# Attention and two MLPs on one Trainium2 core: the projections of queries and keys as one float32 matmul per half head

## What is computed

```python
q_bits = (einsum('bhsd,dk->bhsk', q, proj) > 0)      # proj: 64 x 6
k_bits = (einsum('bhsd,dk->bhsk', k, proj) > 0)
mask = bucket(q_bits)[:, :, :, None] == bucket(k_bits)[:, :, None, :]
scores = where(mask, q @ k.T / 8, -1e9)
x = softmax(scores) @ v                              # 1536 x 512 after the heads are joined
g = s * relu(x @ w_in) ** 2 + b                      # 512 -> 2048
x = g @ w_out
out = ((x @ w1) * (x @ w2) @ w3) @ w_out2            # 512 -> 1024 -> 512
```

## Time and profile before

| | |
|---|---|
| median of three runs | 818.06 us |
| the profiled execution | 818.39 us |
| its span | 816.5 us |
| PE busy | 778.7 us, 95% |
| DVE busy | 481.5 us, 59% |
| ACT busy | 383.7 us, 47% |
| POOL busy | 232.4 us, 28% |
| attention | until about 303 us |
| granted TensorE clock | 1.00 throughout |

### The profile page before, as it was taken

How to read it: one execution, slowest core, us unless ns; L and a number is a source line. 1 busy time by engine, 2 the same in 40 slices (tenths; PEclk the granted TensorE clock), 3 DMA queues, 4 the chain that set the end, 5 groups by cost and what they waited for, 6 DMA issues and landing times.

```text
span 816.5 us, 11692 instructions
## 1 busy us (share of the span) xinstructions
PE 778.7 (95%) x3776; PEld 632.6 (77%) x3776; DVE 481.5 (59%) x838; ACT 383.7 (47%) x718; POOL 232.4 (28%) x150
## 2 busy tenths in 40 slices
PE   3999999999989879999999999999999999999998
PEld 2787778777777768888888888888887888888886
DVE  4899999999989961156665656656576211210220
ACT  2788889888889963344231232323143211211221
POOL 3345555545565454563220211202022000000000
PEclk9999999999999999999999999999999999999999
DMA  5342223232242122233110101101010000001001
GB/s 147 75 97 62 64 61 80 79 81 63 61 119 71 44 78 65 90 103 104 52 51 1 52 0 51 51 1 51 1 53 0 1 26 26 1 14 39 0 0 51
DMA packets 14095, 42.17 MB, mean 52 GB/s; under 512 B 2386, under 2 KB 4434, under 8 KB 14066
## 3 DMA queue, kind: packets, MB, share of 16 engines
q1 hardware_dynamic: 14066, 41.79, 17.9%
HBM read 34.61 MB, written 3.15 MB: 46 GB/s over the span
## 4 chain that ended last, share of the span: by engine, by line
PE 73%; DVE 11%; issue 7%; ACT 5%; DMA 1%; DVEq 0%; SPq 0%; POOL 0%; ACTq 0%
PE psum L984 53%; PE psum L1071 8%; DVE top L728 4%; PE psum L910 3%; PE psum L923 3%; DVE pt_lo L742 3%; ACT prob L501 2%; PE psum L899 2%; PE psum L893 2%; ACT pt_hi L524 1%; DVE x_lo L846 1%; DVE exp_at L735 1%; DMA stage<-in_w_out 1%; PE psum L884 1%; DVE qm L721 1%
## 5 line engine op out<-in xcount | busy, mean ns | idle before, releaser
L501 ACT ACTIVATE prob<-psum,exp_at 128x768 f32<-128x768 f32 x96 | 96.5, 1005 | 29.8 <-DVE exp_at L735 29.8
L742 DVE TENSOR_TENSOR pt_lo<-psum,pt_hi 128x384 fp32r<-128x384 f32 x192 | 98.1, 552 | 11.1 <-ACT pt_hi L524 9.6
L728 DVE TENSOR_REDUCE top<-psum 128x1 f32<-128x768 f32 x96 | 91.0, 948 | 4.3 <-PE psum L899 4.0
L618 ACT ACTIVATE relu<-psum 128x512 f32<-128x512 f32 x48 | 28.6, 597 | 137.3 <-PE psum L984 137.3
L910 PE MATMUL psum<-ident,prob 128*128 128x128 f32 x576 | 85.1, 281 | 7.3 <-DVE pt_lo L742 6.9
L984 PE MATMUL psum<-x_hi,w_c 128*128 128x512 f32 (+1 forms) x288 | 90.6, 396 | 0.0
L984 PE MATMUL psum<-x_hi,w_b 128*128 128x512 f32 (+1 forms) x288 | 90.6, 396 | 0.0
L524 ACT ACTIVATE pt_hi<-psum 128x384 fp32r<-128x384 f32 x192 | 84.2, 495 | 11.0 <-PE psum L910 10.1
L869 DVE TENSOR_TENSOR ab<-psum,a_sb 128x512 f32<-128x512 f32 x24 | 16.6, 692 | 121.3 <-ACT a_sb L668 121.3
L823 DVE SCALAR_TENSOR_TENSOR relu<-psum,relu 128x512 f32<-128x512 f32 x48 | 33.1, 690 | 87.8 <-ACT relu L618 82.7
L910 PEld LDWEIGHTS psum<-ident,prob 128*128 128x128 f32 x576 | 65.4, 141 | 22.1 <-DVE pt_lo L742 13.2
(11 more groups left out here) (92 smaller groups left out, 1516.7 us busy)
## 6 DMA issues: line engine op xcount, KB each, us to landing
raw<-in_qk SPq DMA_DIRECT2D x30, 384.0 KB, 5.0
stage<-in_w_out SPq DMA_DIRECT2D x12, 512.0 KB, 3.4
stage<-in_w3t SPq DMA_DIRECT2D x8, 512.0 KB, 3.2
stage<-in_w_in SPq DMA_DIRECT2D x8, 512.0 KB, 3.3
stage<-in_w SPq DMA_DIRECT2D x8, 512.0 KB, 3.2
raw_v<-in_v SPq DMA_DIRECT2D x16, 192.0 KB, 2.6
qm<-both_hi SPq DMA_DIRECT2D x16, 192.0 KB, 2.7
out<-out_sb SPq DMA_DIRECT2D x12, 256.0 KB, 2.0
```

The costliest lines, as they stand in the source:

```text
L501: act.activation(prob[:, t % 3], score[t % 2], ACT.Exp, bias=exp_at[:, t % 2, 1:2], scale=exp_at[:, t % 2, 0:1], accum_out=rsum[:, (t // 3 ...
L728: dve.tensor_reduce(top[:, t % 2, 1:2], score[t % 2], AX.X, ALU.max, negate=True).then_inc(top_done, 1)
L742: dve.tensor_tensor(pt_lo[at], turned[part].rearrange("p (j q) -> p j q", j=3), pt_hi[at].bitcast(F32), ALU.subtract).then_inc(pt_lo_done, 1)
```

## The change

Queries and keys are loaded a third time, without any scaling or rounding: `qk_f` holds q of a head in its lower 64 partitions and k in its upper 64, two DMAs of 192 KB a head, two heads in turn. `pw` becomes one 128 x 128 float32 matrix, with proj in the rows of q at the columns 64 and 76, and in the rows of k at the columns 96 and 102, where the four rounded ones had it. `dots` is then one plain float32 matmul of 128 rows, 128 columns and 384 positions. It waits for the load instead of q_lo and k_lo; the waits for these two move to the first scores of a head. At the start proj comes first, as two DMAs, then `qk_f` of head 0, and `pw` is four copies on DVE ahead of the scale of head 0; `pj_hi` and `pj_lo` go. `qk_f` of head h + 3 is loaded behind `copy_bits` of head h + 1. The scratch space for DMA descriptors is set to 1024 bytes, which makes room in SBUF.

```diff
-            pw = sb("pw", [P, 4, P], FR, a)
-            pj_lo = sb("pj_lo", [P, BITS], FR, a)
-            pj_hi = sb("pj_hi", [P, BITS], FR, a)
+            pw = sb("pw", [P, P], F32, a)
+            qk_f = sb("qk_f", [P, 2, SEQ], F32, a)
...
+            def load_qk_f(h, par):
+                for w in range(2):
+                    sp.dma_start(qk_f[HALVES[w], par],
+                                 qk[bass.ds(h, 1), :, w].rearrange("o d n -> (o d) n")).then_inc(qk_f_in[par], 16)
...
             for rows in HALVES:
+                sp.dma_start(pj[rows, :], proj).then_inc(proj_in, 16)
+            load_qk_f(0, 0)
+            for rows in HALVES:
                 sp.dma_start(raw[rows, 0, 0], qk[0, :, 0]).then_inc(first_q_in, 16)
-            sp.dma_start(pj[:, :],
-                         proj.unsqueeze(0).broadcast_to([2, HD, BITS])).then_inc(proj_in, 16)
             for rows in HALVES:
                 sp.dma_start(raw[rows, 0, 1], qk[0, :, 1]).then_inc(qk_in[0], 16)
             load_qk(1, 1)
+            load_qk_f(1, 1)
...
             copy_bits(0, 0)
+            load_qk_f(2, 0)
             load_qk(2, 0)
...
                         copy_bits(h + 1, 1 - k)
+                    if not (last or (before_last and k == 1)):
+                        load_qk_f(h + 3, 1 - k)
                     if not last:
                         copy_q_hi(h + 2, k)
...
-            act.wait_ge(proj_in, 16)
-            act.activation(pj_hi[:, :], pj[:, :], ACT.Copy).then_inc(pj_hi_done, 1)
...
+            dve.wait_ge(pw_clear, 1)
+            dve.wait_ge(proj_in, 32)
+            for rows, col in ((HALVES[0], 64), (HALVES[0], 76), (HALVES[1], 96), (HALVES[1], 102)):
+                dve.tensor_copy(pw[rows, col:col + BITS], pj[rows, :]).then_inc(pw_done, 1)
             scale_q(first_q_in, 0)
...
-                pe.matmul(m_ps, pw[:, 0], both_hi[:, par, 0, at], start=True, stop=False)
-                pe.matmul(m_ps, pw[:, 1], both_hi[:, par, 0, at], start=False, stop=False)
-                pe.matmul(m_ps, pw[:, 2], both_hi[:, par, 1, at], start=False, stop=False)
-                pe.matmul(m_ps, pw[0:HD, 3], km[0:HD, par, at], start=False, stop=True).then_inc(dots_done, 1)
+                pe.matmul(m_ps, pw[:, :], qk_f[:, par, at], start=True, stop=True).then_inc(dots_done, 1)
...
+                if i == 0:
+                    pe.wait_ge(q_lo_done, h + 1)
+                    pe.wait_ge(k_lo_done, h + 1)
...
                         if t % 6 == 0:
-                            pe.wait_ge(q_lo_done, h + 2)
-                            pe.wait_ge(k_lo_done, h + 2)
+                            pe.wait_ge(qk_f_in[1 - k], 32 * (pr + k + 1))
                             after(pe, r_copied, 2 * h)
...
-    nc = bacc.Bacc("TRN2", target_bir_lowering=False, num_devices=1)
+    nc = bacc.Bacc("TRN2", target_bir_lowering=False, num_devices=1, dynamic_dma_scratch_size=1024)
```

More of the change, by code:

```diff
@@ L141, in attention_mlp @@
         v_in = [sem("v_in0"), sem("v_in1")]
+        qk_f_in = [sem("qk_f_in0"), sem("qk_f_in1")]
         proj_in = sem("proj_in")
@@ L144, in attention_mlp @@
         rows_set = sem("rows_set")
-        pj_hi_done = sem("pj_hi_done")
-        pj_lo_done = sem("pj_lo_done")
         pw_clear = sem("pw_clear")
@@ L255, in _, with pair @@
             load_qk(3, 1)
-            def pair(pr, last=False):
+            def pair(pr, last=False, before_last=False):
                 for k in range(2):
@@ L277, in _ @@
                 copy_bits(h + 1, 1 - k)
+                if k == 0:
+                    load_qk_f(h + 3, 1)
                 copy_q_hi(h + 2, k)
@@ L693, in k_lo @@
                                   ALU.subtract).then_inc(k_lo_done, 1)
-            dve.memset(pw[:, :, :].bitcast(F32), 0.0).then_inc(pw_clear, 1)
+            dve.memset(pw[:, :], 0.0).then_inc(pw_clear, 1)
             dve.memset(bit_weight[64:96, :], 1.0).then_inc(pw_done, 1)
             dve.memset(top[:, :, 0:1], 1.0).then_inc(pw_done, 1)
+            dve.wait_ge(pw_clear, 1)
+            dve.wait_ge(proj_in, 32)
+            for rows, col in ((HALVES[0], 64), (HALVES[0], 76), (HALVES[1], 96), (HALVES[1], 102)):
+                dve.tensor_copy(pw[rows, col:col + BITS], pj[rows, :]).then_inc(pw_done, 1)
             scale_q(first_q_in, 0)
[L700 to L710, removed]
             dve.wait_ge(rows_set, CONSTANTS)
@@ L936, in _ @@
             pe.wait_ge(rows_set, CONSTANTS)
-            pe.wait_ge(pw_done, 12)
-            pe.wait_ge(q_lo_done, 1)
-            pe.wait_ge(k_lo_done, 1)
+            pe.wait_ge(pw_done, 6)
+            pe.wait_ge(qk_f_in[0], 32)
             dots(0, 0, 0)
```

## The result

| | before | changed |
|---|---|---|
| median, us | 818.21 (6 runs, 816.32 to 820.34) | 824.86 (6 runs, 823.63 to 826.78) |
| ratio, 95% interval | | 1.0078 [1.0057, 1.0099] |
| profiled execution / its span, us | 818.39 / 816.5 | 825.25 / 823.4 |

The account below looks back on a forecast made before the run. DVE and ACT, not PE, were taken to set attention's pace, with slack on PE. 818.06 + 1.2 (start) + 4.1 (three stalls at tile t = 3) = 823.4 us; range 817.0 to 827.0 us.

Parts of the forecast that it names:

- the likeliest case: Whole kernel: later start and a stall at tile t = 3 in three more turns; 823.4 us, slower, chance 0.42.
- Projection on PE: Each projection in attention: one float32 matmul of 0.70 us replaces 1.11 us, saving 0.41 us, 13 us of PE work.
- four products: New projection matmul: float32 accuracy needs four products, so 4 x 0.175 = 0.70 us, with weight loads hidden.
- the 0.22 us: Four matmuls behind the old projection's 64-row pass: 0.93 us instead of 0.71, a cost the change would remove.
- the 13 that I named as a sign: Sign over the whole kernel: PE's busy time about 13 us lower.
- What it is worth in attention: Shorter projections in attention save directly nothing, since DVE runs without a gap; ten places on the chain are near ties.
- Rival 2: Attention: PE bounds after all; ten projections give 4.1 us, 815.2 us, all 30 would give 807.0; faster, chance 0.14.
- The stall at t = 3: Loop turns 3 to 5: earlier PE lets POOL's q_lo start before DVE's exp_at and hold it; 1.38 us each, +4.1 us.
- Rival 1: Loop turns 3 to 5: the stall stays escaped, only the start counts; 819.3 us, the same, chance 0.27.
- The start: Before the first scores: the bit rows' copy goes later behind added loads; +1.2 us, bounds -0.3 and +1.9.
- I take 1.7: At the start: raw of head 1 lands 1.7 us later, from three more issues and 393 KB ahead of it.
- Extra DMA in the loop: Loop: two more load issues of some 0.55 us per head on SP, covered by slack; 0 us.

Follow-up runs that it names:

- the POOL waits: POOL waits for exp_at before q_lo and x_low, added to both kernels: changed kernel 809.84 us, ratio 0.9866; kernel before 809.33 us, ratio 0.9856.
- the third dummy: Changed kernel with three instead of two overwritten extra matmuls ahead of each projection from head 1 on: 821.22 us, against 824.91 us with two.
- the load alone: Kernel before plus the third load of q and k, used by nobody, and the 1024-byte descriptor scratch: 822.57 us, ratio 1.0039.
- the missing pass: Kernel before without the second of the projection's four passes (q with the low part of proj): 823.53 us, ratio 1.0035.
- With proj behind: Changed kernel with the two loads of proj issued behind the first qk_f loads of head 0: 824.09 us, ratio 1.0055.

## Why the prediction was right, and where it was wrong

- **Forecast and range.** 823.4 us, 817 to 827; it came to 824.86, and slower, as the likeliest case had it.
- **Projection on PE.** 0.70 us and a saving of 0.41 were forecast; measured are 0.65 at the one place where it can be read alone, and savings of 0.27 to 0.46. The "four products" estimate was right in size. What was not right everywhere is the 0.22 us that I gave to the matmuls behind the 64-row pass: at t = 6 the four `weighted` ones take 0.78 us (149.02 to 149.80) behind the new matmul too, and not 0.71. PE's busy time fell by 5.1 us instead of the 13 that I named as a sign. Even with turns of one length in both kernels (the POOL waits) it fell by 0.56 us a turn. Where that gap comes from is open. The busy time was a poor sign to name: the third dummy added 30 matmuls to PE, and its busy time went from 780.0 to 779.4 us. The ends of matmuls in a trace are modelled, and start-to-start times are the better sign.
- **What it is worth in attention: directly nothing.** Right for the loop: with the large stalls out, both kernels have turns of 33.4 us. Wrong in turn 0, where the saving is worth 0.3 us: three of the ten places where the chain went over a projection lie before 60 us, and in that stretch PE was the bound and not a near tie. Rival 2 had priced all ten at 4.1 us and falls.
- **The stall at t = 3.** Right in mechanism and size: turns 3, 4 and 5, POOL ahead by 0.04 to 0.05 us, +4.3 us for +4.1. Rival 1 falls. The size rests on a pattern that is partly luck: in the trace before, three turns of six had escaped, and with the load alone it was turns 2, 4 and 6 that escaped. That PE's lateness is what decided it is shown from both sides, by the third dummy (faster with more work) and the missing pass (slower with less).
- **The start: +1.2 forecast, +3.1 measured.** This is the term that failed. The step was "I take 1.7" for raw of head 1, from three issues more and 393 KB more ahead of it; the bounds of the whole term were -0.3 and +1.9. DVE's scale, which waits for that load, started 3.65 us later (14.23 against 10.58). The step priced the load of proj, moved to the front of the queues, as an issue like any other. With proj behind, raw lands at 12.15, 1.6 later than before, and the copy goes 1.08 later: that is what the step had priced, and it was right for it. The other 2.06 us it did not know of. The steps behind it held: 1.65 us were taken for the second projection of the start, and it took 1.66.
- **The first turns.** I had put no number on them. One stall of 1.37 us at 26.50 vanished, another came in turn 1, and 0.6 us went otherwise; that they cancelled is luck. The start's miss of 1.9 was made smaller by the 0.4 of the MLP, so the sum came out only 1.5 us low by the medians.
- **Extra DMA in the loop: 0.** Consistent with the load alone, whose turns have no other length than stalls explain. It may still have moved which turns stall.
- **Left open:** why the kernel before is stalled in turns 1, 2 and 6 and not in 3 to 5, that is, how the phase moves from turn to turn, and whether its other executions, 813.28 to 825.24 us in one group of runs, differ in their stalls; and which resource sets the 33.4 us of a turn without stalls, where DVE, PE and ACT are busy for 31.5, 31.3 and 30.1.

## What to carry to other kernels

Where two engines meet within 0.05 us of each other at every turn, a saving anywhere upstream can cost more than it saves; look for tiny instructions with an odd long duration, and write the order down with a semaphore: here three waits on POOL, which had time to spare, gave 11 us, and a projection shorter by 0.27 to 0.46 us gave 0.3 us at one place and next to nothing elsewhere. Then look again, since the waits made a smaller stall of their own. When a transfer is moved to the head of a queue, ask what it keeps the queue from doing, and not only what its issue costs. And an experiment that adds work to a suspected engine is as telling as one that takes work away.

## What the runs showed of the hardware that I had not expected

- **Small rows at the head of the queues.** Two loads of 64 rows with 6 numbers each held the start of all traffic: 3 GB/s in the third microsecond against 212 with 384 KB in front of them, and a load issued 4.5 us later landed 2.06 us later.
- **A small copy behind large loads.** 54 KB took 6.14 us while loads filled the DMA engines and 2.35 otherwise. Being ready early was worth less than half of what the issue time promised.
- **A tiny instruction behind a POOL subtraction.** An exp_at of 128x2 took 0.16 us when it started 0.04 us before POOL's, and 1.80 us when it started 0.04 to 0.05 us behind it: it ended with POOL's.
- **A float32 matmul leaves two records** of 0.486 us that overlap, so its duration in a group says neither what one costs (0.65 us at 27.39) nor what it saves.
